# Sums over the keys as three fp32r products, and x stored pair by pair

## The chip, the cores and the metric

The kernel runs on one core of a Trainium2 chip. The metric is the device time of one execution in microseconds (us), the median of several runs. The core has five engines with a program each: TensorE (PE, with its weight loader PEld), VectorE (DVE), ScalarE (ACT), GpSimd (POOL) and SyncE (SP). They meet only at semaphores. DMA transfers are issued from the queues of SP, ACT and POOL.

## What is computed

Three stages follow each other. Attention comes first, with 8 batches of 8 heads, 576 tokens and 64 values a head, in fp32:

```python
def phi(x):
    proj = np.einsum('bhsd,df->bhsf', x, w_phi)            # 128 features
    proj = proj - np.max(np.abs(proj), axis=-1, keepdims=True)
    return np.concatenate([np.exp(proj), np.exp(-proj)], axis=-1)
q_p, k_p = (phi(q), phi(k))
kv = np.einsum('bhsf,bhsd->bhfd', k_p, v)                  # sums over the keys
z = np.sum(k_p, axis=2)
num = np.einsum('bhsf,bhfd->bhsd', q_p, kv)
den = np.einsum('bhsf,bhf->bhs', q_p, z)[..., None] + 1e-06
```

Its quotient, as 4608 rows of 512 values, goes through two layers that send each token to one of 8 experts (512 to 1024, relu, back to 512, times a gate). Both choose the expert by an argmax over 8 logits, so small errors can send a token elsewhere. The kernel therefore works in fp32, or in fp32r with a high and a low part: three products (high by high, high by low, low by high) for one.

## The kernel before

Attention runs over 32 pairs of heads (i = 0 to 31). Tokens of a head lie in 4 tiles of 128 and a tail of 64; the tails of both heads of a pair share one tile, on lanes 0 to 63 and 64 to 127. For a pair the kernel transposes k and q (p_t), projects them with w_phi (p_pr), subtracts the largest absolute value (shift_k, shift_q on DVE, into dk and dq), takes exp and exp of the negative of dk (exp_k on ACT, L527 and L528, into kp), and transposes dq before exp_q does the same for q. gather_kv (L1044 to L1062) multiplies v by kp over the tokens for each head: one matmul over the 64 lanes of the tail (L1056) and four over 128 lanes (L1060), 256 columns each, with v and a column of ones as the 65 columns of weights. Both heads write p_k. ACT evicts p_k into kvt at once (evict_kvt, L507), spread_kv transposes it and multiplies the gate's weights in (L1072), ACT evicts that (L511), and numerator (L1115) applies it to qp. divide on DVE writes the quotients into xo, which has two buffers of a whole batch; SP stores a batch of x after its eighth head (L315, L316).

The order on each engine is written out by hand. On TensorE iteration i is: project_k(i) and the tails (L1007, L1027), spread_kv(i-1) (L1072), transpose_k(i+1) (L987), numerator(i-1, 0) (L1115), project_q(i) (L1007), numerator(i-1, 1), transpose_q(i+1) (L997, L999), gather_kv(i, 0), transpose_dq(i) (L1037, L1042), gather_kv(i, 1). On ACT: evict_kvt(i-1), evict_kvs(i-1), evict_xk(i+1) (L517), exp_k(i), evict_xq(i+1) (L521 for p_t, L522 for the tails), exp_q(i) (L532 to L535). On DVE: shift_k(i) and shift_tails(i), divide(i-1, 0), in every fourth iteration locate, then shift_q(i) (L656, L658), divide(i-1, 1), and in every fourth choose. pick_second comes once, in iteration 29.

GpSimd first splits the four pieces of the first expert's weights (a DMA for the high part, a subtraction, L385, for the low one), and then places the tokens of each batch with indirect DMAs (L407) once DVE's locate has their rows. SP loads q, k and v of pair i + 2 in its iteration i (three buffers; it waits for transpose_q and gather_kv of the pair that had the buffer), and after the loop the weights of the second expert and the last batch of x.

Of the kernel before, what the change touches and what calls it, by code (L numbers as in the profile page):

```python
# [29 lines left out]
XG = 5  # L30
NY = 3
# [51 lines left out]
def build(nc, q, k, v, w_phi, modality, w_gate1, bias1, w1a, w2a, w_gate2, w_out2, w1b, w2b, const, out):  # L83
# [8 lines left out]
    with ctx:  # L92
# [68 lines left out]
        with ExitStack() as a:  # L161
            sb("below", [P, 2 * WSET], c=a)
            cst1 = sb("cst1", [P, CW1], c=a)
            zrow = sb("zrow", [1, D], c=a)
            nobody = sb("nobody", [P, E * CAP // P, 2], i32, c=a)
# [3 lines left out]
            xo = [sb(f"xo{n}", [P, CT, D], c=a) for n in range(2)]  # L169
# [6 lines left out]
            dk = sb("dk", [P, 9, FEAT], c=a)  # L176
# [4 lines left out]
            kp = sb("kp", [P, 9, 2 * FEAT], c=a)  # L181
            qp = sb("qp", [P, 2, 9 * P], c=a)
            kvt = sb("kvt", [VW, 4 * FEAT], c=a)
# [39 lines left out]
        s_xst = [sem(f"s_xst{n}") for n in range(2)]  # L223
# [10 lines left out]
        s_max = sem("s_max")  # L234
        s_dk, s_dq, s_dt = sem("s_dk"), sem("s_dq"), sem("s_dt")
        s_kexp, s_qexp = sem("s_kexp"), sem("s_qexp")
        s_c, s_half = sem("s_c"), sem("s_half")
# [30 lines left out]
        def x_rows_main(b):  # L268
            return x_dram[b * S:b * S + MAIN * P, :].rearrange("(p c) d -> p c d", p=P)

# [18 lines left out]
        def _(eng):  # L289
# [23 lines left out]
            def store_x(b):  # L313
                eng.wait_ge(s_xo, H * (b + 1))
                eng.dma_start(x_rows_main(b), xo[b % 2][:, 0:MAIN, :]).then_inc(s_xst[b % 2], 16)  # L315
                eng.dma_start(x_dram[b * S + MAIN * P:(b + 1) * S, :],  # L316
                              xo[b % 2][0:TAIL, MAIN, :]).then_inc(s_xst[b % 2], 16)
# [11 lines left out]
            second_reg = [ctx.enter_context(eng.register(f"second{L}")) for L in range(2)]  # L329
            sets_reg = ctx.enter_context(eng.register("sets_sp"))  # L330

            def load_second(L):
                eng.wait_ge(s_sets, L + 1)
                eng.load(second_reg[L], second[L][0:1, 0:1])
                e = eng.snap(second_reg[L])
                for i in range(PPS):
                    eng.wait_ge(s_low[L][i], 1)
                    raw_load(eng, L, e, i, s_raw[L][i])

            load_second(0)  # L340
            store_x(B - 1)

# [15 lines left out]
        def _(eng):  # L358
# [28 lines left out]
            for i in range(PPS):  # L387
                high_start(i)
                if i:
                    low(i - 1)  # L390
            low(PPS - 1)
# [9 lines left out]
            eng.wait_ge(s_zero, 64)  # L401
            for b in range(B):
                eng.wait_ge(s_idx1, b + 1)
                for c in range(CT):
# [3 lines left out]
                                           pair1[0:m, t, :], None).then_inc(s_bin[0], 16)  # L408

            for L in range(2):  # L410
# [19 lines left out]
                if L == 0:  # L430
                    for r in range(2):
                        eng.wait_ge(s_xst[r], 32 * B // 2)
# [27 lines left out]
        def _(eng):  # L460
# [44 lines left out]
            def evict_kvt(i):  # L505
                eng.wait_ge(s_kv, i + 1)
                eng.activation(kvt[:, :], p_k[0:VW, :], ACT.Copy).then_inc(s_kvt, 1)  # L507
# [43 lines left out]
            for i in range(PAIRS + 1):  # L551
                if i < 3:
                    router_loads((0, 2, 1)[i])
                if i:
                    evict_kvt(i - 1)
                    evict_kvs(i - 1)
# [6 lines left out]
                if i + 1 < PAIRS:  # L563
                    evict_xq(i + 1)
                if i < PAIRS:
                    exp_q(i)
# [706 lines left out]
```

## Time and profile before

| | us |
|---|---|
| median of 3 runs | 1691.74 (1688.46 to 1692.02) |
| the profiled execution | 1688.16 |
| its span | 1686.4 |
| TensorE busy in the span | 1582.9 (94%) |
| DVE, ACT, GpSimd busy | 736.2, 536.5, 364.1 |

Attention fills the first 530 us or so of the span, the first layer of experts runs from there to about 1130 us, and the second to the end. The granted clock of TensorE over the span is 0.971 of full speed. Busy time counts what an engine's instructions took from start to end. Matmuls overlap each other, so the rate of a group is read from the distance between starts, not from the mean duration. A matmul of fp32 operands stands in the trace as two.

### The profile page before, as it was taken

Reading aid. Unit: us, or ns where it says so; the run is one execution under the profiler, and the core shown is the slowest. Engines: PE = TensorE matmul, PEld = TensorE weight load, DVE = VectorE, ACT = ScalarE, POOL = GpSimd, SP = SyncE. Lnnn points to the kernel's source line nnn. Section 1 sums busy time; section 2 is a strip of 40 time slices with the busy share of each in tenths; the row PEclk is TensorE's granted clock in tenths of the full one; section 3 lists DMA queues with packets and bytes.
Section 4 is the critical chain, followed back from the end, with each engine's and each line's share of the span. In section 5 each row is a group of like instructions: output and inputs, shape, how many; then the busy total and the mean of one; then the engine's idle time right before and its main releaser. Section 6 shows DMA issues by size and latency. Waiting matters only on the chain. (4 is left out here: it accounts for less than half of the span.)

```text
span 1686.4 us, 31533 instructions
## 1 busy us (share of the span) xinstructions
PE 1582.9 (94%) x9435; PEld 1294.5 (77%) x9435; DVE 736.2 (44%) x1484; ACT 536.5 (32%) x828; POOL 364.1 (22%) x371
## 2 busy tenths in 40 slices
PE   7999999999995799999999999974999999999996
PEld 5777777777774588888888888763888888888875
DVE  3556456456456343332344233456424223444444
ACT  3444444444441332121232222232313112233233
POOL 1410010010012123223332333125222222222211
PEclk9999999999998799999999999976999999999998
DMA  7633233233250233111113111163224111423243
GB/s 196 170 78 92 57 79 92 57 79 92 57 157 29 82 133 101 38 39 39 39 64 108 42 42 39 36 209 131 87 90 151 39 49 38 141 96 135 93 138 120
DMA packets 166528, 149.88 MB, mean 89 GB/s; under 512 B 130635, under 2 KB 131019, under 8 KB 164816
## 3 DMA queue, kind: packets, MB, share of 16 engines
q1 hardware_dynamic: 125376, 54.92, 12.1%
q0 software_dynamic: 19968, 46.40, 8.6%
q10 hardware_dynamic: 21008, 46.24, 7.9%
q8 instruction: 108, 1.77, 0.5%
q14 instruction: 68, 0.56, 0.2%
HBM read 114.32 MB, written 32.66 MB: 87 GB/s over the span
## 5 line engine op out<-in xcount | busy, mean ns | idle before, releaser
L1154 PE MATMUL bank<-wts,xh 128*128 x640 | 260.3, 407 | 21.1 <-issue 7.5
L1164 PE MATMUL bank<-wts,hh 128*128 x640 | 258.0, 403 | 1.8 <-DVE hl L958 1.6
L1156 PE MATMUL bank<-wts,xl 128*128 x640 | 253.7, 396 | 0.0
L1155 PE MATMUL bank<-wts,xh 128*128 x640 | 253.3, 396 | 0.0
L1166 PE MATMUL bank<-wts,hl 128*128 x640 | 250.6, 392 | 0.0
L1165 PE MATMUL bank<-wts,hh 128*128 x640 | 249.8, 390 | 0.0
L612 ACT ACTIVATE hh<-bank 128x512 fp32r<-128x512 f32 x172 | 93.7, 595 | 342.8 <-PE bank L1251 342.8
L929 DVE TENSOR_SCALAR hid<-bank 128x512 f32<-128x512 f32 x86 | 59.4, 691 | 269.9 <-PE bank L1156 260.7
L1115 PE MATMUL p_n<-kvs,qp 128*128 128x100 f32 (+1 forms) x1280 | 160.9, 276 | 3.1 <-ACT kvs L511 1.0
L1154 PEld LDWEIGHTS bank<-wts,xh 128*128 128x128 f32 x640 | 122.6, 192 | 46.8 <-issue 23.0
L1115 PEld LDWEIGHTS p_n<-kvs,qp 128*128 128x128 f32 (+1 forms) x1280 | 142.3, 180 | 20.6 <-ACT kvs L511 10.5
L952 DVE TENSOR_SCALAR ys<-bank,pair 128x512 f32<-128x512 f32 x86 | 64.5, 750 | 213.7 <-PE bank L1166 212.0
L1156 PEld LDWEIGHTS bank<-wts,xl 128*128 128x128 f32 x640 | 122.1, 191 | 26.4
L1155 PEld LDWEIGHTS bank<-wts,xh 128*128 128x128 f32 x640 | 122.4, 191 | 24.0
L1166 PEld LDWEIGHTS bank<-wts,hl 128*128 128x128 f32 x640 | 120.3, 188 | 26.7
L1164 PEld LDWEIGHTS bank<-wts,hh 128*128 128x128 f32 x640 | 120.5, 188 | 25.2 <-issue 2.7
L1165 PEld LDWEIGHTS bank<-wts,hh 128*128 128x128 f32 x640 | 120.7, 189 | 23.6 <-issue 0.5
L958 DVE TENSOR_TENSOR hl<-bank,hh 128x512 fp32r<-128x512 f32 x172 | 110.9, 685 | 50.3 <-ACT hh L612 50.2
L407 POOL DMA_INDIRECT bins<-pair,idx x40 | 38.5, 963 | 429.9 <-DVE pair L752 420.1
L443 POOL DMA_INDIRECT y_tokens<-ys,pair x43 | 43.3, 1006 | 393.6 <-DVE ys L952 388.3
L656 DVE TENSOR_REDUCE mk<-p_pr 128x8 f32<-128x1024 f32 x32 | 39.2, 1225 | 198.1 <-PE p_pr L1007 193.8
L1060 PE MATMUL p_k<-kp,vs 128*65 128x256 f32 x512 | 124.3, 386 | 0.0
(217 smaller groups left out, 2209.8 us busy)
## 6 DMA issues: line engine op xcount, KB each, us to landing
raw<-in_moe_w ACTq DMA_DIRECT2D x44, 1024.0 KB, 6.4
raw<-in_moe_w SPq DMA_DIRECT2D x16, 1024.0 KB, 7.0
qs<-in_q SPq DMA_DIRECT2D x64, 128.0 KB
ks<-in_k SPq DMA_DIRECT2D x64, 128.0 KB
vs<-in_v SPq DMA_DIRECT2D x64, 128.0 KB
x_tokens<-xo SPq DMA_DIRECT2D x8, 1024.0 KB, 4.1
wts<-raw POOLq DMA_DIRECT2D x4, 1024.0 KB, 6.4
pair<-bins,rowi POOLq DMA_INDIRECT x86
```

The source lines that it names most:

```text
L612: eng.activation(hh[:, half * 4:half * 4 + 4, :].rearrange("p a n -> p (a n)"), src[:, :], ACT.Copy).then_inc(s_hh, 1)
L929: eng.tensor_scalar(hid[:, F // 2:F], b_hb[:, :], 0.0, None, ALU.max).then_inc(s_rb, 1)
L952: eng.tensor_scalar(ys[m % NY][:, :], b_y[:, :], pair2[:, m, 1:2].bitcast(f32), None, ALU.mult).then_inc(s_y, 1)
L958: eng.tensor_tensor(hl[:, part, :].rearrange("p a n -> p (a n)"), src[:, :], hh[:, part, :].rearrange("p a n -> p (a n)").bitcast(f32), AL ...
L1060: last = eng.matmul(o, vs[r][:, 4 * h + c, :], kp[:, 4 * h + c, :], start=False, stop=c == MAIN - 1)
L1115: last = eng.matmul(p_n[h][0:m, c * NW:(c + 1) * NW], qp[:, g, cols], kvs[:, h, g, :], start=g == 0, stop=g == 1)
L1154: eng.matmul(dst[:, :], xh[:, c, :], wh, start=c == 0, stop=False)
L1155: eng.matmul(dst[:, :], xh[:, c, :], wl, start=False, stop=False)
L1156: last = eng.matmul(dst[:, :], xl[:, c, :], wh, start=False, stop=c == DC - 1)
L1164: eng.matmul(b_y[:, :], hh[:, c, :], wh, start=c == 0, stop=False)
L1165: eng.matmul(b_y[:, :], hh[:, c, :], wl, start=False, stop=False)
L1166: last = eng.matmul(b_y[:, :], hl[:, c, :], wh, start=False, stop=c == FC - 1)
```

## The change

- gather_kv runs on high and low parts in fp32r. ACT writes exp_k twice, once as fp32r (kh) and once as fp32 (kp), in two parts of 5 and 4 tiles; DVE's low_k subtracts them into kl, one part ahead of divide(i-1, 1) and one behind it. GpSimd's split_v makes vh (65 columns) and vl (64 columns) of v.
- Head 0 is summed in p_k and head 1 in p_t. Both tails run in head 0's part, after its four tiles, for each of the three products. gather_kv(i, 0) now waits for the eviction of xq(i+1), as p_t holds those transposes. kvt is evicted in two halves.
- x is stored in pairs of heads from three buffers of 128 columns.
- GpSimd runs split_v(i) in a loop over the pairs, with the split of the first weights and the placing of batches between. SP's loads wait for s_vs (split_v) in place of s_kv, and the loads of the second expert's weights move into iteration 30 of its loop, ahead of the last stores.
- zrow and nobody lie inside qp, so ACT waits for their DMAs ahead of the first exp_q.

```diff
@@ SP @@
                 if i >= 3:
                     eng.wait_ge(s_tq, i - 2)
-                    eng.wait_ge(s_kv, i - 2)
+                    eng.wait_ge(s_vs, i - 2)
...
+            def store_x(i):
...
+                b, h = divmod(2 * i, H)
+                cols = slice(h * DH, (h + 2) * DH)
+                r = i % NXO
+                eng.wait_ge(s_xo, 2 * (i + 1))
+                eng.dma_start(x_dram[b * S:b * S + MAIN * P, cols].rearrange("(p c) d -> p c d", p=P),
+                              xo[r][:, 0:MAIN, :]).then_inc(s_xst[r], 16)
+                eng.dma_start(x_dram[b * S + MAIN * P:(b + 1) * S, cols],
+                              xo[r][0:TAIL, MAIN, :]).then_inc(s_xst[r], 16)
...
-                if i % PPB == 0 and i:
-                    store_x(i // PPB - 1)
+                if i == PAIRS - 2:
+                    load_second(0)
+                if i >= 2:
+                    store_x(i - 2)
+            store_x(PAIRS - 2)
+            store_x(PAIRS - 1)
@@ GpSimd @@
+            def split_v(i):
+
+                r = i % 3
+                eng.wait_ge(s_load[r], 16 * 12 * (i // 3 + 1))
                 if i:
-                    low(i - 1)
-            low(PPS - 1)
+                    eng.wait_ge(s_kv, 2 * i)
+                eng.tensor_copy(vh[:, :, :], vs[r][:, :, :]).then_inc(s_vh, 1)
+                eng.wait_ge(s_vh, i + 1)
+                eng.tensor_tensor(vl[:, :, :], vs[r][:, :, 0:DH], vh[:, :, 0:DH].bitcast(f32), ALU.subtract
+                                  ).then_inc(s_vs, 1)
...
+            for i in range(PAIRS):
+                split_v(i)
+                if 1 <= i <= PPS:
+                    high_start(i - 1)
+                if 2 <= i <= PPS + 1:
+                    low(i - 2)
+                if i % PPB == 1 and i > 1:
+                    place_batch(i // PPB - 1)
+            place_batch(B - 1)
@@ ACT @@
-                eng.activation(kp[:, :, 0:FEAT], dk[:, :, :], ACT.Exp)
-                eng.activation(kp[:, :, FEAT:2 * FEAT], dk[:, :, :], ACT.Exp, scale=-1.0).then_inc(s_kexp, 1)
+                if i:
+                    eng.wait_ge(s_kl, 2 * i)
+                for part in (slice(0, 5), slice(5, 9)):
+                    for dst, done in ((kh, s_kh), (kp, s_kexp)):
+                        eng.activation(dst[:, part, 0:FEAT], dk[:, part, :], ACT.Exp)
+                        eng.activation(dst[:, part, FEAT:2 * FEAT], dk[:, part, :], ACT.Exp, scale=-1.0
+                                       ).then_inc(done, 1)
...
                 if i < PAIRS:
+                    evict_kvt(i, 0)
                     exp_q(i)
@@ DVE @@
+            def low_k(i, h):
+                part = (slice(0, 5), slice(5, 9))[h]
+                eng.wait_ge(s_kexp, 2 * i + h + 1)
+                eng.tensor_tensor(kl[:, part, :], kp[:, part, :], kh[:, part, :].bitcast(f32), ALU.subtract
+                                  ).then_inc(s_kl, 1)
...
                 if i < PAIRS:
                     shift_q(i)
+                    low_k(i, 0)
                 if i:
                     divide(i - 1, 1)
+                if i < PAIRS:
+                    low_k(i, 1)
@@ TensorE @@
             def gather_kv(i, h):
-                r = i % 3
+
+                dst = [bank[0:VW, 0:2 * FEAT] for bank in (p_k, p_t)]
+                first = 2 * i + h + 1
                 if h == 0:
-                    eng.wait_ge(s_kexp, i + 1)
+                    eng.wait_ge(s_vs, i + 1)
...
+                    if i + 1 < PAIRS:
+                        eng.wait_ge(s_xq, i + 2)
+                eng.wait_ge(s_kh, first)
+                for m, (v_, k_) in enumerate(((vh, kh), (vl, kh), (vh, kl))):
+                    o = [d[0:v_.shape[2], :] for d in dst]
+                    if m == 2:
+                        eng.wait_ge(s_kl, first)
+                    for c in range(MAIN):
+                        last = eng.matmul(o[h], v_[:, 4 * h + c, :], k_[:, 5 * h + c, :],
+                                          start=m == 0 and c == 0 and h == 0, stop=m == 2 and c == MAIN - 1 and h == 1)
+                    for g in range(2 if h == 0 else 0):
+                        lanes = slice(TAIL * g, TAIL * g + TAIL)
+                        last = eng.matmul(o[g], v_[lanes, 8, :], k_[lanes, MAIN, :],
+                                          start=m == 0 and g == 1, stop=m == 2 and g == 0)
```

## Rows read from the trace of the kernel before

**Rows 1.** Busy us of each engine (instructions) in three stretches; then PEclk, DMA share, GB/s.

```profile
100.00:500.00 400.00, 397.51 (x3142) 309.44 (x3139) 216.35 (x497) 174.88 (x282) 33.50 (x35) 1.00 0.33 83
500.00:550.00 50.00, 27.13 (x200) 20.50 (x198) 26.91 (x104) 9.88 (x17) 9.97 (x11) 0.82 0.09 32
600.00:1100.00 500.00, 497.33 (x2670) 421.57 (x2668) 176.87 (x401) 123.26 (x211) 141.87 (x144) 1.00 0.18 58
```

**Rows 2.** Timeline, one period: start us, us, engine, line, [idle before <-releaser]; TensorE.

```profile
308.81 0.60 PE L999 MATMUL p_t<-cst,qs 128*128 128x128 f32 x4
...
309.34 0.19 PEld L1056 LDWEIGHTS p_k<-kp,vs 64*65 64x65 f32 x2 [0.17 <-issue]
309.34 0.64 PE L1056 MATMUL p_k<-kp,vs 64*65 64x256 f32 x2
...
309.91 1.49 PEld L1060 LDWEIGHTS p_k<-kp,vs 128*65 128x65 f32 x8 [0.38 <-issue]
309.91 1.94 PE L1060 MATMUL p_k<-kp,vs 128*65 128x256 f32 x8
...
311.69 1.04 PE L1037 MATMUL p_c<-cst,dq 128*128 128x128 f32 x8
...
312.56 0.27 PE L1042 MATMUL p_n<-cst,dq 128*128 128x128 f32 x1
...
315.21 1.16 PE L1007 MATMUL p_pr<-wphi,xk 64*128 64x128 f32 x16
```

**Rows 3.** The same timeline, ACT and DVE.

```profile
299.53 0.59 ACT L507 ACTIVATE kvt<-p_k 65x512 f32<-65x512 f32 x1 [0.17 <-PE p_k L1060]
...
304.19 1.17 ACT L527 ACTIVATE kp<-dk 128x1152 f32<-128x1152 f32 x1 [1.05 <-DVE dq L677]
...
305.26 1.15 ACT L528 ACTIVATE kp<-dk 128x1152 f32<-128x1152 f32 x1
...
307.49 1.23 DVE L658 TENSOR_TENSOR dq<-p_pr,mq 128x1024 f32<-128x1024 f32 x1
...
309.44 0.60 ACT L521 ACTIVATE xq<-p_t 128x512 f32<-128x512 f32 x1 [3.04 <-PE p_t L999]
...
309.94 0.36 ACT L522 ACTIVATE xtt<-p_n 64x256 f32<-64x256 f32 x1
...
312.87 1.02 ACT L532 ACTIVATE qp<-p_c 128x1024 f32<-128x1024 f32 x1 [2.57 <-PE p_n L1042]
...
315.32 0.59 ACT L507 ACTIVATE kvt<-p_k 65x512 f32<-65x512 f32 x1 [0.17 <-PE p_k L1060]
```

**Rows 4.** Groups by form, 100 to 500 us: busy us, mean ns | idle before.

```profile
L1060 PE MATMUL p_k<-kp,vs 128*65 128x256 f32 x400 | 97.1, 386 | 0.0
L1060 PEld LDWEIGHTS p_k<-kp,vs 128*65 128x65 f32 x400 | 50.9, 137 | 42.7 <-issue 19.2
...
L1115 PEld LDWEIGHTS p_n<-kvs,qp 128*64 128x64 f32 x204 | 18.5, 136 | 5.0
...
L1056 PEld LDWEIGHTS p_k<-kp,vs 64*65 64x65 f32 x100 | 9.5, 132 | 8.4 <-issue 8.4
```

**Rows 5.** Timeline, first layer of experts: fp32r matmuls of 512 columns.

```profile
902.69 0.39 PE L1155 MATMUL bank<-wts,xh 128*128 x1
...
902.91 0.39 PE L1156 MATMUL bank<-wts,xl 128*128 x1
```

**Rows 6.** Groups of the whole span: subtractions of two SBUF operands on DVE and GpSimd.

```profile
L385 POOL TENSOR_TENSOR wts<-raw,wts 128x2048 fp32r<-128x2048 f32 x4 | 18.1, 4536 | 4.2 <-DMA wts<-raw 4.1
...
L639 DVE TENSOR_TENSOR wts<-raw,wts 128x2048 fp32r<-128x2048 f32 x4 | 9.0, 2285 | 0.1
```

**Rows 7.** Timeline, pair 0.

```profile
21.93 1.15 ACT L527 ACTIVATE kp<-dk 128x1152 f32<-128x1152 f32 x1
...
24.26 0.19 PEld L1056 LDWEIGHTS p_k<-kp,vs 64*65 64x65 f32 x2 [0.17 <-ACT kp L528]
```

**Rows 8.** Timeline, a pair with locate ahead of shift_q.

```profile
292.71 1.23 DVE L658 TENSOR_TENSOR dq<-p_pr,mq 128x1024 f32<-128x1024 f32 x1
...
294.15 0.36 ACT L522 ACTIVATE xtt<-p_n 64x256 f32<-64x256 f32 x1
```

More of the change, by code:

```diff
@@ L30 @@
 XG = 5
+NXO = 3
 NY = 3
@@ L222, in build @@
         s_load = [sem(f"s_load{n}") for n in range(3)]
-        s_xst = [sem(f"s_xst{n}") for n in range(2)]
+        s_xst = [sem(f"s_xst{n}") for n in range(NXO)]
         s_raw = [[sem(f"s_raw{l}_{n}") for n in range(PPS)] for l in range(2)]
@@ L311, in load, with load_second @@
                                       s_[t, MAIN * P:S, :]).then_inc(s_load[r], 16)
[L313 to L317, printed above, removed]
+            def store_x(i):
[7 more added lines that the diff above has]
+                              xo[r][0:TAIL, MAIN, :]).then_inc(s_xst[r], 16)
+            second_reg = [ctx.enter_context(eng.register(f"second{L}")) for L in range(2)]
+            def load_second(L):
+                eng.wait_ge(s_sets, L + 1)
+                eng.load(second_reg[L], second[L][0:1, 0:1])
+                e = eng.snap(second_reg[L])
+                for i in range(PPS):
+                    eng.wait_ge(s_low[L][i], 1)
+                    raw_load(eng, L, e, i, s_raw[L][i])
             load(0)
@@ L399, in place_group, with place_batch @@
                                            ).then_inc(s_bin[1], 16)
-            eng.wait_ge(s_zero, 64)
-            for b in range(B):
+            def place_batch(b):
                 eng.wait_ge(s_idx1, b + 1)
@@ L430, in _ @@
                 if L == 0:
-                    for r in range(2):
-                        eng.wait_ge(s_xst[r], 32 * B // 2)
+                    for r in range(NXO):
+                        eng.wait_ge(s_xst[r], 32 * len(range(r, PAIRS, NXO)))
                 else:
@@ L503, in router_loads, with evict_kvt @@
                                   ).then_inc(s_misc, 16)
-            def evict_kvt(i):
-                eng.wait_ge(s_kv, i + 1)
-                eng.activation(kvt[:, :], p_k[0:VW, :], ACT.Copy).then_inc(s_kvt, 1)
+            def evict_kvt(i, h):
+                eng.wait_ge(s_kv, 2 * i + h + 1)
+                eng.activation(kvt[:, 2 * h * FEAT:2 * (h + 1) * FEAT], (p_k, p_t)[h][0:VW, 0:2 * FEAT], ACT.Copy
+                               ).then_inc(s_kvt, 1)
             def evict_kvs(i):
@@ L1051, in gather_kv @@
                         eng.wait_ge(s_set, 1)
-                o = p_k[0:VW, 2 * h * FEAT:2 * (h + 1) * FEAT]
-                lanes = slice(TAIL * h, TAIL * h + TAIL)
-                if h == 1:
-                    eng.wait_ge(s_half, i + 1)
-                tail = eng.matmul(o, vs[r][lanes, 8, :], kp[lanes, 8, :], start=True, stop=False)
-                if h == 0:
-                    tail.then_inc(s_half, 1)
-                for c in range(MAIN):
-                    last = eng.matmul(o, vs[r][:, 4 * h + c, :], kp[:, 4 * h + c, :], start=False, stop=c == MAIN - 1)
+                    if i + 1 < PAIRS:
[12 more added lines that the diff above has]
+                                          start=m == 0 and g == 1, stop=m == 2 and g == 0)
+                        if g == 0 and m == 2:
+                            last.then_inc(s_kv, 1)
                 if h == 1:
```

57 lines of the change are left out of this document (26 added, 31 removed).

## The prediction

> **What bounds the kernel now.** I read the stages first. Over 100 to 500 us TensorE is busy 397.5 of 400 us at the full granted clock, ACT 175, DVE 216, GpSimd 34; the later stages, which the change does not touch, are busy nearly as much [rows 1]. So attention is set by TensorE's order of work, and any gap that the change opens there is paid in full. The second view is one pair of heads in order of time. Two evictions of kvt start at 299.53 and 315.32: a period of 15.79 us, 32 of them [rows 3]. In it I look for what TensorE does between the q transposes and the next projection, and for how early ACT and DVE are with what it needs then [rows 2, 3]. The third view keeps shapes apart and shows idle time of the weight loader where the shape of the stationary tile changes [rows 4].
>
> **The products themselves.** Today one half of gather_kv starts at 309.34 (weights) and the dq transposes follow at 311.69: 2.35 us. The other half lies between the last dq transpose, 312.56, and the weights of the next projection, 315.21: 2.65 us [rows 2]. Each fp32 product stands in the trace as two matmuls: sixteen of 128 rows and four of 64. The eight of L1060 end with a start at 309.91 + 1.94 - 0.38 = 311.47, and the next tile starts 0.22 later, so one of 256 columns takes 0.215 us [rows 2]. After the change there are 30 fp32r matmuls of 256 columns. The fp32r matmuls of 512 columns later in the kernel start 0.23 us apart [rows 5]: 0.213 for the columns if they go at the rate of the 0.215 above (two matmuls of 256 each), and some 0.014 over. Bounds for 256 columns are therefore half of 0.215, 0.108, and 0.107 + 0.014, 0.121; I take 0.114, as neither row is nearer.
>
> **What a change of tile shape costs.** L1056 works on 64 rows, L1060 on 128. The second L1056 matmul starts at 309.34 + 0.64 - 0.38 = 309.60, and the first of L1060, counted back from 311.69 by eight times 0.2155, at 309.97: 0.36 apart instead of 0.215, so the change of rows costs 0.15 us. The loader shows it: its next load starts at 309.91, 0.09 us after the last column has gone in (309.60 + 0.215), and 65 columns of weights take 0.055 more (309.97) [rows 2, 4]. numerator's tail does the same where the stationary tile goes from 128 columns to 64: 5.0 us of idle loader in 51 changes, 0.10 each [rows 4]. The new gather has more such changes than the old. Head 0 runs, for each of the three products, four matmuls of 128 rows and then the two tails of 64 rows; the low part of v has 64 columns instead of 65. That is five changes inside head 0's part and one on the way to the dq transposes (0.20, since 128 columns load there); in head 1's part two, from 65 to 64 columns and back. The two tails of a product lie in different rows and different banks, and projections in such a form run two at a time (the 16 matmuls of 128 columns from 315.21 start within 1.16 - 0.27 us, 0.06 each [rows 2]), so I count a pair once, 0.12; serial they would cost 0.114 more each.
>
> Sum for head 0: 0.055 + 12 x 0.114 + 3 x 0.12 + 5 x 0.15 + 0.20 = 2.73 us, against 2.35: +0.38. Head 1: 0.11 + 12 x 0.114 + 2 x 0.15 + 0.09 = 1.87, against 2.65: -0.78. Of the products alone the change gains 0.40 us a pair.
>
> The Trainium skill, TensorEngine Tiling (Array Packing), Gotcha 1, says that different row tiles can't use one PSUM bank at the same time. The kernel before agrees as far as it goes (its row-tiled projections fill two banks in parallel), and the changed code puts head 1 into p_t for the same reason; were the tails to run serially after all, the sum would be 32 x 0.34 = 11 us longer.
>
> **The wait that this brings.** p_t also holds the transposes of the next pair's q. gather_kv of head 0 must now wait until ACT has evicted them and the tails. Today that eviction runs from 309.44 to 309.94 + 0.36 = 310.30 and lies under gather_kv, which started at 309.34 [rows 2, 3]. The new start is 310.30 + 0.05 = 310.35: +1.01 us, and behind it on TensorE stands everything else of the pair. Nothing else can fill it, as TensorE takes its work in order.
>
> **ACT.** exp_k writes kp twice, as 8 instructions for 2. L527 to L528 is 1.07 us for 1152 elements, L521 to L522 0.50 us for 512 [rows 3]; from these, 640 elements take 0.61 to 0.64 and 512 take 0.50 to 0.54, so 4.4 to 4.7 us for 2.3. It starts at 304.19 and ends by 308.6 to 309.0, ahead of the transposes at 309.44: hidden, with 0.4 us to spare. With 0.2 us instead of 0.1 beside each instruction's elements it would end at 309.6 and cost 0.2 us a pair. The kvt eviction is split; head 0's falls into the wait for the dq transposes, head 1's follows exp_q and is due at the spread 1.5 us after the projection's start: hidden by about 0.4 us.
>
> **DVE and GpSimd.** low_k subtracts 1280 and 1024 elements. The nearest row is a subtraction of 2048 of the same kind, 2.29 us [rows 6], so 1.48 and 1.22 us. dq is ready at 307.49 + 1.23 = 308.72; low_k(0) ends near 310.2 and is needed, by the sum above, 1.7 us after 310.35: hidden. low_k(1) comes after divide and ends near 312.5, needed near 316. GpSimd splits v: 2048 elements take it 4.54 us [rows 6], so 576 to 585 take about 1.3 each, 2.6 us in a period of which 11 are free. In seven pairs locate comes ahead of shift_q: dq's subtraction starts at 292.71, 1.45 us before ACT's second eviction at 294.15 [rows 8]; low_k(0) then ends near 295.4 and is needed at 296.3: still hidden, and the indirect DMAs of place_batch run beside it. Pair 29 has pick_second as well: up to 1 us once.
>
> The Trainium skill, GPSIMD Engine Reference, section 8, says that GpSimd contends for SBUF with DVE instructions of two SBUF inputs; low_k is one. No row here has the two side by side. Twice the time for low_k(0) in those seven pairs would make the sum about 0.5 us x 7 = 3 us longer.
>
> **Stores and queues.** x leaves in 32 stores of a quarter of the size, with 512-byte pieces. DMA is busy 0.33 in this stage [rows 1], the slots are reused three pairs later, and the last store, a quarter as large, is issued as soon as the last quotient is there, as before: nothing, at worst 1 us. On SP each load is now issued earlier (after split_v, not after gather_kv), so nothing waits for it.
>
> **First and last pair.** In pair 0 exp_k starts only at 21.93, and gather_kv at 24.26 [rows 7]. exp_k of 4.4 to 4.7 us and the evictions (0.86) put it at 27.5: +3.3, with the sum above +2.9 us. The last pair has no q to wait for: -0.4.
>
> **Sum.** 30 x (1.01 + 0.38 - 0.78 = +0.61) = +18.3; +2.9 - 0.4: +20.8 us. The profiled execution took 1688.16 us (span 1686.4), which gives 1709.0. The runs shown lie at 1688.46, 1691.74 and 1692.02; the profiled one is at their low end, so I take 1690 as the level: 1711 us.
>
> **Rivals.**
> - *Faster: the tile changes inside gather_kv are not paid.* If the loader went over them as it does within a group, head 0 would take 1.78 us and head 1 1.57, and a pair 1.01 - 0.57 - 1.08 = -0.64. 30 of them make -19, while the first pair (+1.7) and the last (-1.7) cancel: about 1671 us. For it: 65 and 128 columns follow each other without a gap (L1060 to L1037). Against it: the gap stands behind every one of the 64-row groups and 64-column tails [rows 4]. It decides once more than four of the eight changes go unpaid (0.61 / 0.15). 0.12.
> - *It cancels:* matmuls at 0.108, no cost for 65 to 64 columns, and a shorter wait by 0.1: within 3 us of before. 0.08.
> - *ACT is late:* exp_k ends after the transposes, 0.2 to 0.5 us a pair on top: 1717 to 1727. For it only 0.4 us of cover. 0.12.
> - *The change doesn't do what it says:* fp32r of 256 columns costs what a fp32 matmul of 256 does, 0.215. 30 of them make +3 us a pair: about 1800. Against it [rows 5]. 0.03.
> - *The clock:* a gap of 1 us in each period lets the granted clock fall; after 18.9 us of idle it is 0.82 over 500 to 550 us [rows 1]. No row has a gap of 1 us in the midst of dense work. Some 10 us or more on top; 0.03.
> - *The forecast*, 0.62. Its own bounds: 0.108 to 0.121 a matmul (-6 to +7), tails serial (+11), no cost from 65 to 64 (-9): 1697 to 1727.
>
> **Chances.** Slower by over 0.2% (3.4 us, about what a measurement can tell from no change): 0.62 + 0.12 + 0.03 + 0.03 = 0.80. Within 0.2%: 0.08. Faster: 0.12. The range, 1689 to 1727, leaves out the faster rival, the fp32r rival and most of the clock's, under 0.2.
>
> **What the next profile should show.** ahead of the first matmul of gather_kv a wait of TensorE for ACT's xtt of about 1 us; fp32r matmuls 0.11 to 0.12 apart; loader gaps of 0.1 to 0.3 us at each tail; a period of 16.4 us; exp_k ending before the q transposes. Tails without gaps, or a period under 15.8 us, would prove me wrong; an idle of ACT of zero ahead of L521 would show the cover of exp_k gone.

## The result

| | before | after |
|---|---|---|
| median | 1691.88 us (1688.46 to 1693.77, 4 runs) | 1713.66 us (1708.23 to 1714.38, 4 runs) |
| profiled execution, its span | 1688.16, 1686.4 | 1713.97, 1712.1 |
| period of a pair (median over the pairs) | 15.79 | 16.27 |

The changed kernel takes 1.0124 times as long as the kernel before (95% interval 1.0098 to 1.015). Slower was forecast, at 1711 us. The attention stage shows where it came from. Two windows of the changed kernel follow; the columns are those of [rows 1].

```profile
0.00:50.00 50.00, 33.99 (x225) 27.56 (x225) 18.56 (x26) 20.10 (x44) 9.73 (x27) 0.83 0.74 193
100.00:500.00 400.00, 370.56 (x3311) 315.22 (x3310) 269.02 (x524) 233.75 (x451) 94.64 (x81) 1.00 0.31 72
```

From 100 to 500 us TensorE is busy 27 us less than in [rows 1] and yet does less of attention in that time. So it stands idle, 27 us more in some 24.5 periods. The groups by form of the same stretch (busy us, mean ns | idle before, and what released the engine) say where:

```profile
L1105 PE MATMUL p_k<-kh,vh 128*65 128x256 f32 x96 | 15.6, 284 | 27.7 <-ACT xtt L546 20.7 <-issue 7.0
...
L1167 PEld LDWEIGHTS p_n<-kvs,qp 128*64 128x64 f32 x196 | 17.8, 136 | 4.8
```

Nearly all of TensorE's idle time (27.7 of 29.4 us) lies ahead of the first matmul of gather_kv(i, 0), 1.15 us in each of 24 groups. For 20.7 us of it the profile names ACT's eviction of xtt as what ended it; for 7.0 us, six groups of the same length, it names nothing ("issue"). The timeline of one period (columns as in [rows 2]) shows the new order of TensorE:

```profile
306.04 0.60 PE L1042 MATMUL p_t<-cst,qs 128*128 128x128 f32 x4
...
307.76 0.43 PEld L1105 LDWEIGHTS p_k<-kh,vh 128*65 128x65 f32 x4 [1.36 <-issue]
307.79 0.66 PE L1105 MATMUL p_k<-kh,vh 128*65 128x256 f32 x4 [1.15 <-issue]
...
308.38 0.13 PEld L1109 LDWEIGHTS p_k<-kh,vh 64*65 64x65 f32 x1 [0.19 <-issue]
308.38 0.33 PE L1109 MATMUL p_k<-kh,vh 64*65 64x256 f32 x1
...
308.38 0.33 PE L1109 MATMUL p_t<-kh,vh 64*65 64x256 f32 x1
...
308.64 0.69 PE L1105 MATMUL p_k<-kh,vl 128*64 128x256 f32 x4
...
309.26 0.33 PE L1109 MATMUL p_k<-kh,vl 64*64 64x256 f32 x1
...
310.39 1.09 PE L1080 MATMUL p_c<-cst,dq 128*128 128x128 f32 x8
...
311.32 0.27 PE L1085 MATMUL p_n<-cst,dq 128*128 128x128 f32 x1
...
311.35 0.70 PE L1105 MATMUL p_t<-kh,vh 128*65 128x256 f32 x4
...
311.89 0.63 PE L1105 MATMUL p_t<-kh,vl 128*64 128x256 f32 x4
...
312.36 0.63 PE L1105 MATMUL p_t<-kl,vh 128*65 128x256 f32 x4
...
312.93 1.16 PE L1050 MATMUL p_pr<-wphi,xk 64*128 64x128 f32 x16
```

and the same period on ACT and DVE:

```profile
305.25 0.61 ACT L556 ACTIVATE kp<-dk 128x512 f32<-128x512 f32 x1
...
306.68 0.60 ACT L545 ACTIVATE xq<-p_t 128x512 f32<-128x512 f32 x1 [0.81 <-issue]
306.87 1.48 DVE L706 TENSOR_TENSOR kl<-kp,kh 128x1280 fp32r<-128x1280 f32 x1
307.17 0.36 ACT L546 ACTIVATE xtt<-p_n 64x256 f32<-64x256 f32 x1
```

In these lines lies the whole difference of a period. The shown pair has locate in it, but the four stretches below are the same within 0.02 us in nearly all pairs from the second to the last but one. "Forecast" is the forecast difference.

| from, to | before | after | difference | forecast |
|---|---|---|---|---|
| last q transposes (start of the group) to the first weights of gather_kv | 308.81 to 309.34: 0.53 | 306.04 to 307.76: 1.72 | +1.19 | +1.01 |
| head 0: those weights to the dq transposes | 309.34 to 311.69: 2.35 | 307.76 to 310.39: 2.63 | +0.28 | +0.38 |
| the dq transposes | 311.69 to 312.56: 0.87 | 310.39 to 311.32: 0.93 | +0.06 | 0 |
| head 1: last dq transpose to the next projection | 312.56 to 315.21: 2.65 | 311.32 to 312.93: 1.61 | -1.04 | -0.78 |
| sum | | | +0.49 | +0.61 |

The median period grew by 0.49 us, from 15.786 to 16.274.

### The profile page after: what moved, and what is told of

Same layout as the page of the kernel before. It is cut to its first block and busy times, and to the rows that moved or that the text cites. A ratio compares the mean times of both kernels' runs of the same rounds, so it can differ in the third digit from the quotient of the medians.

```text
span 1712.1 us, 32660 instructions
## 1 busy us (share of the span) xinstructions
PE 1570.4 (92%) x9755; PEld 1320.5 (77%) x9755; DVE 816.7 (48%) x1548; ACT 617.7 (36%) x1052; POOL 441.4 (26%) x435
## 5 line engine op out<-in xcount | busy, mean ns | idle before, releaser
L1167 PE MATMUL p_n<-kvs,qp 128*128 128x100 f32 (+1 forms) x1280 | 162.5, 278 | 3.1 <-ACT kvs L535 1.0
L1167 PEld LDWEIGHTS p_n<-kvs,qp 128*128 128x128 f32 (+1 forms) x1280 | 143.8, 182 | 20.7 <-ACT kvs L535 10.5
L1208 PEld LDWEIGHTS bank<-wts,xl 128*128 128x128 f32 x640 | 122.6, 192 | 26.6
L466 POOL DMA_INDIRECT out<-ys,pair x43 | 43.5, 1011 | 371.7 <-DVE ys L995 371.7
L663 DVE TENSOR_TENSOR wts<-raw,wts 128x2048 f32 x44 | 98.9, 2289 | 56.0 <-ACT wts L493 52.9
L614 ACT ACTIVATE hid<-bank 128x512 f32<-128x512 f32 x86 | 51.4, 598 | 199.2 <-PE bank L1208 190.7
```

The costliest lines, as they stand in the source:

```text
L466: eng.indirect_dma_start(y_dram if L == 0 else out, bass.IndirectOffsetOnAxis(ap=pair2[:, n, 0:1], axis=0), ys[n % NY][:, :], None, bounds ...
L663: eng.tensor_tensor(wts[:, bass.ds(g % 2, 1), 1, cols], raw[:, i, :].unsqueeze(1), wts[:, bass.ds(g % 2, 1), 0, cols].bitcast(f32), ALU.su ...
L1167: last = eng.matmul(p_n[h][0:m, c * NW:(c + 1) * NW], qp[:, g, cols], kvs[:, h, g, :], start=g == 0, stop=g == 1)
L1208: last = eng.matmul(dst[:, :], xl[:, c, :], wh, start=False, stop=c == DC - 1)
```

## The experiments

Periods below are distances between starts of the reduction into mk on DVE, the first instruction of a pair there; the median over the pairs is given.

### The stores alone

```diff
-            xo = [sb(f"xo{n}", [P, CT, D], c=a) for n in range(2)]
+            xo = [sb(f"xo{n}", [P, CT, 2 * DH], c=a) for n in range(NXO)]
...
-                if i % PPB == 0 and i:
-                    store_x(i // PPB - 1)
+                if i == PAIRS - 2:
+                    load_second(0)
+                if i >= 2:
+                    store_x(i - 2)
```

> The kernel before with the stores of x alone changed: 32 stores of two heads from three buffers, and the second weights' loads moved into SP's loop. My theory, by the traces of before and after: the whole of the added time lies on TensorE inside attention, and the stores lie beside it. Period of a pair 15.79 us as before, time within 0.2% of before (about 1692 us). The rival, that 512-byte pieces or the order on SP's queue hold something up, expects part of the 22 us here: 1697 us or more, and waits of DVE for a store or of TensorE for x ahead of the first tile of experts.

Measured: 1687.18 us (1683.75 to 1691.07, 10 runs), ratio 0.9985 (0.9976 to 0.9995) to 1690.52 of the kernel before in the same job (19 runs), and a period of 15.785. The stores cost nothing; the interval even lies just below 1. Of the periods behind the first pair only the last differs, 15.78 instead of 16.63 us. In the trace of the kernel before, exp_q of the pair ahead of it starts 1.9 us late, behind 4.49 us without work on ACT where [rows 3] has 2.57, and the profile names nothing in the core that it waited for:

```profile
489.14 1.02 ACT L532 ACTIVATE qp<-p_c 128x1024 f32<-128x1024 f32 x1 [4.49 <-remote]
```

The fp32 kernel with its tails behind (below) stores x like the kernel before and has no such period: its last one is 15.11 us, as the others. So the long period isn't due to the stores, and its cause stays open. In the trace of the changed kernel a store of 256 KB has landed 2.7 us after its issue (the columns are issues, KB each, median us from issue to landing), where one of four times the size took 4.1, and its slot is wanted three pairs later:

```profile
x_tokens<-xo SPq DMA_DIRECT2D x32, 256.0 KB, 2.7
```

### The wait: for p_t alone

The changed kernel, with a signal of its own from the first of ACT's two evictions:

```diff
-                eng.activation(xq[:, :], p_t[:, :], ACT.Copy)
+                eng.activation(xq[:, :], p_t[:, :], ACT.Copy).then_inc(s_pt, 1)
...
-                        eng.wait_ge(s_xq, i + 2)
+                        eng.wait_ge(s_pt, i + 2)
```

> The changed kernel, but gather_kv waits for the eviction of p_t alone (a semaphore of its own), not for the tails' eviction behind it. Theory: TensorE stands still because of this wait, and every part of it is paid. ACT's second eviction starts 0.50 us after the first and ends 0.26 us later than it, so the wait is shorter by about 0.27 us a pair: period 16.27 to 16.00, time of the changed kernel less 8 us, about 1705 us. The rival, that gather_kv would wait for another engine's work anyway (kh of ACT, vh of GpSimd), expects the period to stay at 16.27 and the wait to be put down to another releaser.

Measured: 1705.41 us (4 runs), ratio 1.0094 (1.0077 to 1.0111) to the kernel before, period 16.013. The period fell by 0.26 us, as expected. In its timeline TensorE starts with the end of L546 (303.15 + 0.36), not 0.26 us after it:

```profile
303.15 0.36 ACT L546 ACTIVATE xtt<-p_n 64x256 f32<-64x256 f32 x1
303.51 0.66 PE L1105 MATMUL p_k<-kh,vh 128*65 128x256 f32 x4 [0.89 <-ACT xq L545]
```

The wait is real and is paid in full: what is taken off it comes off the period.

### The wait: its place among the waits

In the prediction gather_kv started 0.05 us after the eviction's end. In the changed kernel it is 307.76 - (307.17 + 0.36) = 0.23. TensorE has one more wait, for kh, behind this one. Here they change places:

```diff
-                    if i + 1 < PAIRS:
-                        eng.wait_ge(s_xq, i + 2)
                 eng.wait_ge(s_kh, first)
+                if h == 0 and i + 1 < PAIRS:
+                    eng.wait_ge(s_xq, i + 2)
```

> The changed kernel with one thing moved: TensorE waits for ACT's xtt (the evictions of p_t and p_n) as the last of the waits of gather_kv(i, 0) instead of ahead of its wait for kh. The semaphores and everything else are the same. In the changed kernel the weights of the gather start 0.22 us after xtt has ended, where I had put 0.05; kh has long been ready by then. Theory A: the extra 0.17 us is the sequencer going through the waits and weights that stand behind the one that comes last; with that one placed last, the weights start about 0.05 us after xtt's end and the median period falls from 16.27 to about 16.10 us. Theory B: it is the way of the signal from ACT to TensorE, whatever stands behind it; the distance stays at 0.22 and the period at 16.27 us, within 0.03.

The timeline of ACT and of the weight loader:

```profile
305.06 0.36 ACT L546 ACTIVATE xtt<-p_n 64x256 f32<-64x256 f32 x1
305.54 0.43 PEld L1105 LDWEIGHTS p_k<-kh,vh 128*65 128x65 f32 x4 [1.25 <-issue]
```

Measured: period 16.160, which is 0.11 less; 1705.4 us in its one run. The weights start 305.54 - 305.42 = 0.12 us after the eviction. So theory A holds for 0.11 us of the 0.17: that is what the satisfied wait (one whose condition was already met) behind the late one cost. The other 0.06 to 0.07 us stays in both, and no run takes it apart.

### The changes of tile shape

A change of rows is a step on TensorE from a stationary tile (weights) of 128 rows to one of 64, or back. Here are the same matmuls, with the six tails of head 0's part behind its twelve matmuls of 128 rows. Six changes of rows become two.

```diff
+                for m, (v_, k_) in enumerate(((vh, kh), (vl, kh), (vh, kl))):
                     for g in range(2 if h == 0 else 0):
```

> The changed kernel, but in head 0's part the tails of the three products come together, after the twelve matmuls of 128 rows: two changes between 128 and 64 rows instead of six, the same matmuls otherwise. Theory: each change costs 0.147 us (0.264 between the starts instead of 0.117), so four fewer give 0.59 us a pair: period 16.27 to 15.68, 31.4 pairs, about 18.5 us less than the changed kernel, 1695 us. The rival, that the distance belongs to the tails' matmuls themselves (64 rows, two at a time, in two banks) and not to the change, expects 16.27 and 1714 us.

Measured: 1691.69 us (10 runs), ratio 1.0017 (1.0006 to 1.0029), period 15.700 where 15.68 was expected. Four changes of rows less, two in each direction, are worth 16.274 - 15.700 = 0.574 us, 0.144 each, and no other work changed. That the changes inside gather_kv are not paid, the rival that ended faster, is refuted. In its timeline the tails follow each other 0.17 and 0.12 us apart, and two by two:

```profile
297.32 0.64 PE L1105 MATMUL p_k<-kl,vh 128*65 128x256 f32 x4
...
297.89 0.33 PE L1110 MATMUL p_k<-kh,vh 64*65 64x256 f32 x1
297.89 0.33 PE L1110 MATMUL p_t<-kh,vh 64*65 64x256 f32 x1
298.06 0.28 PE L1110 MATMUL p_k<-kh,vl 64*64 64x256 f32 x1
...
298.18 0.28 PE L1110 MATMUL p_k<-kl,vh 64*65 64x256 f32 x1
...
298.39 1.09 PE L1080 MATMUL p_c<-cst,dq 128*128 128x128 f32 x8
```

### Is it the rows, or also the columns?

The numerator's tail has 64 columns of weights among groups of 128. For head 0 it now takes 128, and its result is read from the first 64 lanes as before.

```diff
-                        cols, m = slice(8 * P + TAIL * h, 8 * P + TAIL * h + TAIL), TAIL
+                        m = TAIL if h else P
+                        cols = slice(8 * P + TAIL * h, 8 * P + TAIL * h + m)
```

> The changed kernel, but numerator of head 0 takes all 128 columns of the tail tile as weights (the 64 of head 1 give rows that nothing reads) instead of 64; head 1's numerator stays. Question: what made the weight loader pause before 64 columns there, when the changed gather went from 65 to 64 columns and back without any pause. Theory A (what the prediction held): the pause is that of a change of tile shape, so with 128 columns throughout it is gone at head 0's numerator and stands at head 1's. Theory B: it belongs to the change of output or row range of the tail and stays. The period changes by less than 0.1 us either way; the verdict is read from the loader's gaps.

The groups by form over 100 to 500 us (busy us, mean ns | idle before):

```profile
L1168 PEld LDWEIGHTS p_n<-kvs,qp 128*128 128x128 f32 x900 | 104.2, 192 | 10.7 <-ACT kvs L535 7.6
L1168 PEld LDWEIGHTS p_n<-kvs,qp 128*64 128x64 f32 x100 | 9.1, 136 | 2.4
```

The idle time ahead of the 64-column form halved with its number (4.8 us for 196 instructions, 2.4 for 100), and none came up ahead of the wide form (10.7 us, as in the changed kernel). The period fell to 16.234, 0.04 us less (1707.57 us in its one run). So going from 128 columns to 64 does cost the loader 0.1 us, at equal rows. But from 65 to 64 and back, inside head 1's part, no gap stands: in the timeline of the changed kernel its three products start 0.54 and 0.47 us apart, which is four matmuls at 0.117 each, and 0.07 more at the start of the first. Whether that is because 65 columns are near to 64 or because these are fp32r was not told apart.

### Without the wait

Each head's tails stand behind its own twelve matmuls, in its own bank; head 0 then writes nothing to p_t, and the wait for xq can go.

```diff
-                    if i + 1 < PAIRS:
-                        eng.wait_ge(s_xq, i + 2)
...
+                lanes = slice(TAIL * h, TAIL * h + TAIL)
+                for m, (v_, k_) in enumerate(((vh, kh), (vl, kh), (vh, kl))):
+                    last = eng.matmul(dst[h][0:v_.shape[2], :], v_[lanes, 8, :], k_[lanes, MAIN, :],
+                                      start=False, stop=m == 2)
+                last.then_inc(s_kv, 1)
```

> The changed kernel with each head's three tails behind its own twelve matmuls, head 1 still in p_t, so that nothing of head 0's part needs p_t and its wait for ACT's evictions is gone (head 1's comes after the dq transposes, which wait for the same thing). Theory: from the measured terms, wait -1.19, head 0 four changes fewer -0.59, head 1 three matmuls (+0.35) and one change (+0.15) more: -1.28 us a pair, period 14.99; with the first pair's wait gone as well, about 1713.7 - 40 - 3 = 1670 us, faster than before by 1.2%. The rival, that ACT's, DVE's or GpSimd's new work sets the pace once TensorE is let go, expects a wait for kh, kl, vh or kvt in place of it and a period of 15.5 us or more (1686 us or more).

Measured: 1661.24 us (1655.98 to 1662.34, 4 runs), ratio 0.9824 (0.9804 to 0.9844), period 14.394. The period is 0.6 us better than expected. The timeline shows most of it:

```profile
311.05 0.33 PE L1107 MATMUL p_t<-kh,vh 64*65 64x256 f32 x1
311.06 0.37 PE L1050 MATMUL p_pr<-wphi,xk 64*128 64x128 f32 x1
```

Head 1's tails work on 64 rows, and so do the projections behind them: the two start together, and the 0.35 us for three more matmuls and the 0.15 for a change of rows, both in the expected sum, are not paid. Another 0.17 us come from gather_kv's start, now 0.36 us after the first q transpose (0.53 in the kernel before, whose gather began with 64 rows). But now DVE is late in the pairs in which locate comes ahead of shift_q. TensorE waits for kl:

```profile
277.08 1.48 DVE L706 TENSOR_TENSOR kl<-kp,kh 128x1280 fp32r<-128x1280 f32 x1
...
278.61 0.69 PE L1103 MATMUL p_k<-kl,vh 128*65 128x256 f32 x4 [0.82 <-DVE kl L706]
```

These periods are 15.62 to 15.83 us long, and that of pair 29, with pick_second, 18.6. The cover that hid locate in the changed kernel was the wait: with the tails last and the wait kept, these pairs are at 15.93 to 15.99 us, 0.23 to 0.29 above the median, where the kernel before has 0.24; pair 29, at 17.04, is not covered there.

### With locate behind low_k

The kernel of the last experiment; in those pairs DVE first only reads the ranks out of p_k, and does the rest of locate, and pick_second, behind low_k(i, 1).

```diff
-                    locate(i // PPB - 1)
-                if i == PPB * (B - 1) + 1:
-                    pick_second()
+                    read_rank(i // PPB - 1)
                 if i < PAIRS:
...
                     low_k(i, 1)
+                if i % PPB == 1 and i > 1:
+                    locate(i // PPB - 1)
+                if i == PPB * (B - 1) + 1:
+                    pick_second()
```

> The kernel without the wait (each head's tails behind its twelve matmuls), and DVE's locate behind low_k(i, 1) instead of ahead of shift_q; only its two reads of p_k stay where they were. In the trace of the kernel without the wait every fourth pair takes 15.8 us instead of 14.39, and pair 29 (pick_second) 18.6, with TensorE waiting for low_k of head 0. Theory: this is DVE's queue, and moving about 1 us of locate (and pick_second's 1.7) behind low_k takes nearly all of it away: every fourth pair 14.7 us, time about 1661 - 6 x 1.1 - 3.5 = 1651 us. The rival, that GpSimd's placing of tokens (its indirect DMAs beside DVE's subtraction) causes the long pairs, expects them to stay long, or a new wait for vh.

Measured: 1647.26 us (1645.42 to 1649.9, 4 runs), ratio 0.9746 (0.9727 to 0.9765). The period stays at 14.394 and those pairs are at 14.63 to 14.79. Of the wait for kl 0.5 us is left in the groups by form over 100 to 500 us:

```profile
L1109 PE MATMUL p_k<-kl,vh 128*65 128x256 f32 x108 | 18.4, 292 | 0.5 <-DVE kl L706 0.5
```

Here the indirect DMAs start behind locate and no longer stand beside low_k, so this run alone doesn't tell DVE's order from the rival, the DMAs beside low_k. The trace without the wait does: beside them low_k takes 1.48 and 1.22 us, as in every other pair. This version is faster than both kernels. Its arithmetic is that of the change.

### How much of that is fp32r?

The kernel before, in fp32 and without high and low parts, with each tail behind its head's four matmuls:

```diff
-                tail = eng.matmul(o, vs[r][lanes, 8, :], kp[lanes, 8, :], start=True, stop=False)
-                if h == 0:
-                    tail.then_inc(s_half, 1)
-                for c in range(MAIN):
-                    last = eng.matmul(o, vs[r][:, 4 * h + c, :], kp[:, 4 * h + c, :], start=False, stop=c == MAIN - 1)
+                for c in range(MAIN):
+                    eng.matmul(o, vs[r][:, 4 * h + c, :], kp[:, 4 * h + c, :], start=c == 0, stop=False)
+                if h == 1:
+                    eng.wait_ge(s_half, i + 1)
+                last = eng.matmul(o, vs[r][lanes, 8, :], kp[lanes, 8, :], start=False, stop=True)
+                if h == 0:
+                    last.then_inc(s_half, 1)
```

> The kernel before, fp32 products and all, with one edit: each head's tail behind its four matmuls of 128 rows instead of ahead of them. It tells what of the gain of the kernel without the wait is due to fp32r and what to the order of the tails. Theory: the change of tile shape between a tail and the next projection (both 64 rows) falls away and the two overlap, which in the kernel without the wait gave 0.6 us a pair beyond the sum; head 0's part costs the same as before. Period 15.79 to 15.1, about 1690.5 - 21 = 1670 us. If only the fp32r products made the gain: 15.79 and 1690 us.

Measured: 1671.93 us (4 runs), ratio 0.9889 (0.9872 to 0.9905), period 15.113. In its timeline the last tail again runs beside the projections:

```profile
303.56 0.43 PE L1058 MATMUL p_k<-kp,vs 64*65 64x256 f32 x1
303.57 0.48 PE L1007 MATMUL p_pr<-wphi,xk 64*128 64x128 f32 x2
```

So the order of the tails alone takes the period from 15.79 to 15.11, and the fp32r products, once their order opens no gap, from 15.11 to 14.39: 0.72 us a pair. The changed kernel has the same products and spends more than this on the wait (1.19) and on its six changes of rows (0.146 each).

### The clock in the first pair

The changed kernel's first pair takes 18.58 us, where the kernel before took 13.46. Seven matmuls on constants stand in iteration 0 just ahead of gather_kv(0, 0). Their result is not used.

```diff
+                if i == 0:
+                    for _ in range(7):
+                        eng.matmul(p_c[:, 0:2 * P], c1_("ones"), cst1[:, 0:2 * P], start=True, stop=True)
```

> The changed kernel with seven matmuls of 256 columns that nothing uses in the first pair, where TensorE waits 3.2 us for ACT. In the trace of the changed kernel the first pair takes 18.58 us against 13.46, of which the wait is 3.05; the matmuls behind it stand 0.22 us apart instead of 0.117. Theory: the granted clock falls because of the wait, and with TensorE kept at work there the first pair comes down by about 2 us, to 16.5. The rival, that the clock has not yet risen that early whatever TensorE does, expects 18.6 or more.

The first fence is the timeline of the changed kernel; the second is a window of this one (columns as above) and the third its timeline.

```profile
27.15 0.66 PE L1105 MATMUL p_k<-kh,vh 128*65 128x256 f32 x4 [2.86 <-ACT xtt L546]
...
28.12 1.11 PE L1105 MATMUL p_k<-kh,vl 128*64 128x256 f32 x4
...
31.02 1.97 PE L1080 MATMUL p_c<-cst,dq 128*128 128x128 f32 x8
```

```profile
0.00:50.00 50.00, 37.22 (x270) 30.89 (x270) 18.68 (x27) 22.63 (x49) 10.75 (x29) 0.90 0.77 191
```

```profile
23.73 3.69 PE L1195 MATMUL p_c<-cst 128*128 128x256 f32 x14
27.13 0.76 PE L1105 MATMUL p_k<-kh,vh 128*65 128x256 f32 x4
...
28.07 0.68 PE L1105 MATMUL p_k<-kh,vl 128*64 128x256 f32 x4
```

Measured: the first pair took 15.79 us instead of 18.58, although gather_kv starts at the same time. The period stays at 16.27, and the one run took 1707.23 us. In the changed kernel TensorE stands 2.86 us and the four matmuls of vl then take 1.11 us, the eight dq transposes 1.97; with TensorE kept at work they take 0.68 and, as in the later pairs, 1.1. The rows of the first are at the lower level of the clock (1.2 GHz), those of the second at 2.4 GHz. So 2.8 of the 5.1 us that the first pair lost were the clock, behind the idle time that the wait for ACT made.

Each kernel has one trace here, and the level at this place differs between them. In the trace of the changed kernel the level rose at 24.4 us, fell at 27.8 and rose again at 34.6. With the wait placed last the first four matmuls behind it are slow already (0.66 us in the changed kernel), and so are the q transposes ahead of it (1.06 us for 0.60 at full clock):

```profile
27.49 1.09 PE L1105 MATMUL p_k<-kh,vh 128*65 128x256 f32 x4 [2.67 <-ACT xtt L546]
```

There the level did not fall, it had not risen. What holds over all the traces: in the five with this wait (the changed kernel, the wait for p_t alone, its place, the tails last, the wide tail) TensorE works at the lower level behind it until 31.1 to 34.8 us, and the first pair takes 16.64 to 18.77 us; in the five with TensorE at work there, or waiting 0.9 us at most, it is at the full level for good from 23.7 to 26.6 us on. The kernel without the wait for ACT lies between: there TensorE waits 1.89 us for kl, and the level is low from 27.5 to 30.9 us. So the wait costs clock, but 2.8 us is the difference of two traces, not a fixed price.

## Why the prediction was right, point by point

**The bound.** TensorE's order of work sets attention, and a gap there is paid in full: two experiments took 0.26 and 0.11 us off the wait, and both came off the period in full.

**The wait.** The mechanism was right, and its size 0.18 us too low (1.19 for 1.01). The term at fault is the 0.05 us from the eviction's end to the weights: it was 0.23, of which the wait behind it in the queue is 0.11. What ended it is named as forecast (ACT xtt) for three quarters of it.

**Head 0.** Forecast 2.73 us, measured 2.63. A matmul of 256 columns takes 0.117 us, in the bounds of 0.108 to 0.121. From the tails at 308.38 to those at 309.26 are 0.88 us, where five starts at 0.117 would be 0.585: two changes of rows cost 0.29 us, 0.146 each, as forecast (0.15). With the tails last, where three pairs of tails follow each other, the pieces of a change can be told apart: the first tail starts 0.21 us behind the last matmul of 128 rows, the second 0.17 behind the first, the third 0.12 behind the second (297.89, 298.06, 298.18), and the first dq transpose 0.21 behind that (298.39). So a change costs 0.09 us where it happens and 0.055 on the start behind it, as [rows 2] had it from L1056 to L1060. The exit to the dq transposes cost that as well and not 0.20, and its second piece, 0.06, falls among the dq transposes, where the table has it. Within head 0's part the exit is therefore 0.09 for 0.20, and that is the 0.10 by which the forecast was too high. The two tails of a product start together, into two banks, so counting the pair once held. The Trainium skill, TensorEngine Tiling (Array Packing), Gotcha 1, has it that different row tiles can't use one bank together; the trace fits it, with the tails of L1109 at 308.38 both in p_k and p_t, and no run here puts two row tiles into one bank at the same time.

**Head 1.** Forecast 1.87 us, measured 1.61. The two changes from 65 to 64 columns, 0.15 each in the sum, cost nothing. I had carried them over from the numerator's 128 to 64 columns; the row was right for that change (experiment with the wide tail) and not for this one. It was the largest miss of the period and offset the one in the wait.

**The rival that ended faster** would have needed more than four unpaid changes of shape. The six changes of rows were all paid, the two of columns were not. The rival in which it cancels wanted three things, and only that one of them came.

**ACT and DVE.** exp_k runs from 301.17 to 305.86, 4.69 us, at the upper end of 4.4 to 4.7, and ends ahead of the q transposes: the cover held. low_k takes 1.48 and 1.22 us, to the digit, and was hidden, also behind locate (16.51 us against 16.02 in those pairs, the same half microsecond as elsewhere). That this cover rests on the wait for ACT, the prediction did not say; the kernel without the wait shows it.

**GpSimd.** v's high part took 0.67 us and the low part 1.40, not 1.3 each. The contention with low_k, which the prediction put at up to 3 us, doesn't reach DVE. The timeline of the changed kernel has both sides: L419 beside L706 and by itself.

```profile
306.16 0.98 POOL L419 DMA_INDIRECT bins<-pair,idx  x1 [0.30 <-issue]
...
307.44 1.74 POOL L419 DMA_INDIRECT bins<-pair,idx  x1 [0.30 <-issue]
...
309.20 1.22 DVE L706 TENSOR_TENSOR kl<-kp,kh 128x1024 fp32r<-128x1024 f32 x1
309.49 1.75 POOL L419 DMA_INDIRECT bins<-pair,idx  x1 [0.30 <-issue]
```

These are three of the five indirect DMAs of a batch. GpSimd's 0.98 becomes 1.74 and 1.75 us, while L706 keeps the 1.48 and 1.22 that it takes in every pair. The Trainium skill, GPSIMD Engine Reference, section 8, names the contention between the two engines. The trace agrees, and it is GpSimd that pays here, which has the time. The lines show how: both long ones end 0.83 us after the subtraction beside them (309.18 for 308.35, 311.24 for 310.42), and so do all fourteen such DMAs of the seven batches, 0.78 to 0.84 us after it. A DMA that starts inside the subtraction seems to wait until it is over; one that had started 0.7 us ahead of it (306.16) takes its 0.98 us.

**First and last pair.** Both were missed: +5.1 us for +2.9, and +1.4 for -0.4. In the first pair gather_kv starts 2.9 us later (27.15 for 24.26), where 3.3 was forecast, but the matmuls behind the wait ran at the lower clock, and the prediction took them at the full one. It treated the clock as a rival for the steady pairs, where it stayed at 1.00 with a gap of 1.15 us in each, and not where the wait is long. In the last pair there is no q projection behind gather_kv, so spread_kv meets exp_q on ACT, whose queue holds kvt's second half:

```profile
541.12 1.11 PE L1124 MATMUL p_k<-msel,kvt 65*128 65x73 f32 x8 [1.21 <-ACT kvt L530]
...
542.74 6.55 PE L1167 MATMUL p_n<-kvs,qp 128*128 128x100 f32 x40 [0.51 <-ACT kvs L535]
```

The same two waits in the kernel before:

```profile
521.94 1.11 PE L1072 MATMUL p_k<-msel,kvt 65*128 65x73 f32 x8 [0.68 <-ACT kvt L507]
...
523.56 4.96 PE L1115 MATMUL p_n<-kvs,qp 128*128 128x100 f32 x40 [0.51 <-ACT kvs L511]
```

The wait for kvt is 0.53 us longer; the prediction had both evictions of kvt hidden, which was said for the steady pair only. With it the pair is still 0.17 us shorter than before up to spread_kv, where 0.4 was forecast. The rest, 1.6 us, is the forty matmuls of L1167 that take 6.55 us instead of 4.96, at the lower level of the clock from 543.2 to 546.6. The change did not cause that as far as the traces tell: with the wait placed last and with the tails last, these two waits are the same within 0.01 us and the forty matmuls take 4.96, and in the fp32 kernel with its tails behind, which waits as the kernel before does, they take 8.10. What decides it is not shown.

**The sum.** 28 x 0.49 = 13.7, plus 0.77 in pair 29 (16.02 to 16.79), less 0.35 in the last full period (16.63 to 16.28) are 14.1 us; unrounded, the thirty periods give 14.2, where the forecast had 18.3. Of the 0.77, 0.29 are a longer head 0's part: there TensorE waits for kl behind pick_second. The last full period is shorter only for what held ACT up in the trace before. With 5.1 + 1.4 for the two ends, where the forecast had 2.5, the last quotient comes 20.8 us later by the trace (starts at 549.9 and 529.1). So the forecast's +20.8 was met by terms that missed in both directions, the periods 4.1 us too high and the ends 4.0 too low. That the two agree to the digit is luck, all the more as 1.6 us of the last pair are not of the change. The bounds of the forecast, added up, are 1696 and 1729 us, not 1697 and 1727.

The spans of the profiled executions differ by 25.7 us; the other 5 lie in the two layers of experts, which are 1157.3 us long before and 1162.2 after, with the same work. By the clock records of the two traces TensorE was at the lower level for 101 us of this stretch before and for 113 after; at half the speed, 11.5 us more of it are some 5.7 us, an estimate that covers the difference; no experiment was made on it. The experiments, which leave these layers as they are, have 105 to 119 us at the lower level and 1157.4 to 1161.5 us. The medians of the runs differ by 21.8 us.

## What to carry to other kernels

Before a product is split into more and cheaper ones, list for each piece which buffer it writes and who reads that buffer now: here a tail of half a tile that went into the transposes' bank cost 1.2 us a pair, more than the cheaper products gave. On TensorE group matmuls by the rows they work on, and let a short group of 64 rows stand next to other work of 64 rows: that order alone was worth 1.1% in the kernel before, and with fp32r, without the wait and with locate moved 2.5%. A wait that is taken away uncovers the next engine, so look for what was hidden behind it (DVE's locate), and price first and last pairs by their own neighbours and their own clock.

## What the runs showed of the hardware

- A matmul of 256 fp32r columns takes 0.117 us, and a fp32 one of the same size 0.215.
- Between stationary tiles of 128 and of 64 rows a change costs 0.146 us (0.144 by the experiment), in either direction: the next matmul starts 0.21 us after the last one instead of 0.117, and the one behind it 0.17. From 128 to 64 columns of weights at equal rows, 0.1 us of idle loader; from 65 to 64 in fp32r, none.
- Matmuls of 64 rows of two different kinds, in different banks, run side by side: the tails of a gather and the projections behind it (311.05 and 311.06 us, 303.56 and 303.57 us).
- One satisfied wait on TensorE behind the one that comes last costs 0.11 us.
- GpSimd's work for an indirect DMA that starts during a DVE subtraction of two SBUF operands takes 1.66 to 1.86 us instead of 0.98 and ends 0.78 to 0.84 us after the subtraction; DVE's time doesn't change.
- Behind a wait of 2.67 to 3.01 us in the first pair TensorE worked at the lower clock level until 31.1 to 34.8 us; 1.15 us in every period of 16.27 left it at 1.00.
